# Two heads' last 64 keys as one square tile, and another order of the steps, in a linear-attention and mixing kernel

## The reference

```python
q_p, k_p = phi(q), phi(k)
kv = einsum('bhsf,bhsd->bhfd', k_p, v)      # sum over tokens
z = sum(k_p, axis=2)
out = (q_p @ kv) / (q_p . z + 1e-06)
```

## Time and profile before

| | us |
|---|---|
| median of three runs | 1393.31 |
| the three runs | 1392.87, 1393.31, 1397.05 |
| profiled execution, its own time | 1397.19 |
| its span, first to last instruction | 1395.3 |
| TensorE busy | 1333.8 |
| VectorE busy | 756.6 |
| ScalarE busy | 599.2 |
| mean granted TensorE clock | 0.981 |

### The profile page before, as it was taken

How to read it: one execution, slowest core, us unless ns; L and a number is a source line. 1 busy time by engine, 2 the same in 40 slices (tenths; PEclk the granted TensorE clock), 3 DMA queues, 4 the chain that set the end, 5 groups by cost and what they waited for, 6 DMA issues and landing times. The chain is left out here.

```text
span 1395.3 us, 25154 instructions
## 1 busy us (share of the span) xinstructions
PE 1333.8 (96%) x9720; PEld 1192.8 (85%) x9720; DVE 756.6 (54%) x1275; ACT 599.2 (43%) x1079; POOL 13.1 (1%) x18
## 2 busy tenths in 40 slices
PE   8779999999999999999999999998899999999998
PEld 7559898889888888888888888998798998998997
DVE  6557355545654544644565455451855755754853
ACT  3345445354353533534435344352533443533532
POOL 0000000000000000000000000000300000000000
PEclk9879999999999999999999999999999999999999
DMA  4421202202212111220221221221110110110101
GB/s 136 141 62 41 59 27 79 64 18 80 62 36 71 50 50 42 66 71 15 76 62 37 71 54 50 73 70 48 65 65 31 43 65 31 41 64 32 40 30 38
DMA packets 92657, 78.56 MB, mean 56 GB/s; under 512 B 62736, under 2 KB 71056, under 8 KB 91536
## 3 DMA queue, kind: packets, MB, share of 16 engines
q1 hardware_dynamic: 92560, 77.09, 18.4%
HBM read 57.75 MB, written 19.02 MB: 55 GB/s over the span
## 5 line engine op out<-in xcount | busy, mean ns | idle before, releaser
L459 PE MATMUL psm<-xk_hi,wk_hi 128*128 128x288 f32 x512 | 154.4, 302 | 14.5 <-issue 7.1
L982 PE MATMUL psh<-y_hi,win_hi 128*128 128x288 f32 x512 | 154.8, 302 | 13.4 <-ACT h L1067 9.0
L830 DVE TENSOR_TENSOR k_lo<-square,k_hi 128x288 fp32r<-128x288 f32 x128 | 58.5, 457 | 195.1 <-ACT square L677 194.8
L983 PE MATMUL psh<-y_lo,win_hi 128*128 128x288 f32 x512 | 153.1, 299 | 0.0
L459 PE MATMUL psm<-k_hi,wv_hi 128*128 128x288 f32 x512 | 152.8, 299 | 0.0
L984 PE MATMUL psh<-y_hi,win_lo 128*128 128x288 f32 x512 | 152.5, 298 | 0.0
L459 PE MATMUL psm<-xk_lo,wk_hi 128*128 128x288 f32 x512 | 152.2, 297 | 0.0
L459 PE MATMUL psm<-k_lo,wv_hi 128*128 128x288 f32 x512 | 152.0, 297 | 0.0
L459 PE MATMUL psm<-xk_hi,wk_lo 128*128 128x288 f32 x512 | 151.9, 297 | 0.0
L459 PE MATMUL psm<-k_hi,wv_lo 128*128 128x288 f32 x512 | 151.7, 296 | 0.0
L1125 DVE SCALAR_TENSOR_TENSOR conv<-h,taps,conv 128x576 f32<-128x576 f32 x64 | 55.2, 862 | 143.2 <-ACT conv L1069 143.2
(11 more groups left out here) (130 smaller groups left out, 2900.4 us busy)
## 6 DMA issues: line engine op xcount, KB each, us to landing
v_nat<-in_v SPq DMA_DIRECT2D x32, 320.0 KB, 3.6
qk<-in_q SPq DMA_DIRECT2D x32, 288.0 KB, 3.3
qk<-in_k SPq DMA_DIRECT2D x32, 288.0 KB, 3.7
den<-den_scr SPq DMA_DIRECT2D x64, 144.0 KB, 3.0
y_scr<-y SPq DMA_DIRECT2D x64, 144.0 KB, 2.0
y<-y_scr SPq DMA_DIRECT2D x8, 1152.0 KB, 5.6
out<-rows SPq DMA_DIRECT2D x32, 256.0 KB, 2.0
stage<-in_moe_w_in SPq DMA_DIRECT2D x4, 512.0 KB, 3.2
```

Source lines behind the costliest of these rows:

```text
L459: return nc.tensor.matmul(o, lhsT, rhs, start=first, stop=last, skip_group_check=True)
L830: nc.vector.tensor_tensor(k2_lo[:, i, :], square[:, i % 2, :], k2_hi[:, i, :].bitcast(F32), ALU.subtract).then_inc(k2_lo_ready, 1)
L982: nc.tensor.matmul(o, wh, xh, start=first, stop=False, skip_group_check=True)
L983: nc.tensor.matmul(o, wh, xl, start=False, stop=False, skip_group_check=True)
```

## The change

There are four parts. (1) The tails of both heads' keys become one square tile: the host lays k so that rows 0 to 63 hold head 0's last 64 tokens in columns 512 to 575 and rows 64 to 127 head 1's in columns 576 to 639, with zeros elsewhere, and v so that the tail tile holds head 0's tokens on partitions 0 to 63 and head 1's on 64 to 127. One matmul over 128 rows makes both tails' features, and one of 130 columns an exponential adds both heads' tails to the sums, which now lie as (exponential, head). (2) The second key exponential becomes a step of its own, EL. (3) The order: each batch's E(0) stands ahead of the tiles, RC, DV and the mixing steps stand at fixed places (`BESIDE_NEXT`, `ALONE`), VectorE takes each k_lo one tile later (`vector_order`), and HK and HR move from ScalarE to VectorE. (4) One iteration is taken out of the loop and written out, and pair 0's loads are issued during the iteration before.

```diff
+KEYS = 2 * (TT - 1) + 1
-FILL_NS = {"E": 1600, "QT": 1600, "EK": 3200, "PICK": 3200, "NUM": 1600}
-FIRST_FILL, RC_AFTER, DV_AFTER = 4000, 2500, 8500
+FILL_NS = {"E": 1600, "QT": 1600, "EK": 1600, "EL": 1600, "PICK": 3200, "NUM": 3200}
-    return [(s, p) for p in range(PAIRS) for s in ("E", "QT", "EK", "M", "KV", "PICK", "DEN", "NUM")]
+    return [(s, p) for p in range(PAIRS) for s in ("E", "QT", "EK", "EL", "M", "KV", "PICK", "DEN", "NUM")]
...
-        steps += [("E", p), ("QT", p), ("EK", p)] + before("DEN", "NUM") + [("WARM", p)] + before("RC")
-        steps += [("M", p), ("KV", p), ("PICK", p)] + before("DV")
+        steps += [("E", p), ("QT", p), ("EK", p), ("EL", p)] + ([("DV", p - 2)] if p > 1 else []) + before("DEN", "NUM") + [("WARM", p), ("M", p), ("KV", p)]
+        steps += before("RC") + [("PICK", p)]
     p = PAIRS - 1
-    steps += [("DEN", p), ("NUM", p), ("XK", 2, 0), ("HK", 2, 0), ("LK", 2, 0), ("RC", p)]
-    steps += [("XR", 2, 0), ("HR", 2, 0), ("LR", 2, 0), ("DV", p)]
-    return steps + [(s + w, 2, 1) for w in "KR" for s in "XHL"]
+    steps += [("DV", p - 1), ("DEN", p), ("NUM", p), ("RC", p)] + mixing("K", 2, 0) + mixing("R", 2, 0) + [("DV", p)]
+    return steps + mixing("K", 2, 1) + mixing("R", 2, 1)
...
+BESIDE_NEXT = {
+    ("M", 0): [("XK", 1, 0)],
+    ("QT", 1): [("RC", 0)],
+    ("M", 1): [("HK", 1, 0), ("LK", 1, 0)] + mixing("K", 1, 1) + mixing("R", 1, 0) + mixing("R", 1, 1) + [("DV", 0)],
+    ("QT", 2): [("RC", 1)],
+    ("PICK", 2): [("DV", 1)],
+    ("QT", 3): [("RC", 2)],
+    ("M", 3): [("DV", 2)] + mixing("K", 2, 0) + [("XR", 2, 0)],
+    ("R", 1, 3): [("HR", 2, 0), ("LR", 2, 0)],
+    ("V-", 1, 0): [("RC", 3)],
+    ("V", 1, 1): [("DV", 3)] + mixing("K", 2, 1) + mixing("R", 2, 1),
+}
...
+def vector_order(steps):
+
+    out, tile = [], []
+    for step in steps:
+        if step[0] in ("K", "K+", "R", "V"):
+            out += tile
+            tile = []
+        if step[0] in ("K", "K+"):
+            tile = [step]
+        else:
+            out.append(step)
+    return out + tile
...
-        with eng.Fori(1, LAST) as c:
+        with eng.Fori(1, LAST - 1) as c:
             work((c, 0), (c, 1), iteration(True, True))
+        work((None, LAST - 1), (None, LAST), iteration(True, True))
         work((None, LAST), None, iteration(True, False))
...
+                if kind == "E" and step[1] + 1 == PAIRS and after(a) is not None:
+                    load_qk(0, after(a))
                 if kind == "KV" and step[1] + 1 < PAIRS:
                     load_v(step[1] + 1, a)
+                if kind == "KV" and step[1] + 1 == PAIRS and after(a) is not None:
+                    load_v(0, after(a))
...
-            key_tile(0, TT - 1).then_inc(shared_bank, 1)
+            mm(k_tail(p, a), qk[:, p % 2, 1, P * (TT - 1):P * TT], phi[:], True, True).then_inc(shared_bank, 1)
             feature_chunk(1, 1, True)
             feature_chunk(0, 0, True)
-            await_(pe, shared_bank, 3 * PAIRS, a, 3 * p + 1)
-            key_tile(1, TT - 1).then_inc(shared_bank, 1)
-            key_tile(0, 0)
             key_tile(1, 0)
-            await_(pe, shared_bank, 3 * PAIRS, a, 3 * p + 2)
+            await_(pe, shared_bank, 2 * PAIRS, a, 2 * p + 1)
             feature_chunk(0, 1, True).then_inc(shared_bank, 1)
             key_tile(1, 1)
-            key_tile(0, 1)
-            await_(pe, shared_bank, 3 * PAIRS, a, 3 * p + 3)
+            key_tile(0, 0)
+            await_(pe, shared_bank, 2 * PAIRS, a, 2 * p + 2)
             feature_chunk(1, 0, False).then_inc(raw_features, 1)
-            for t in range(2, TT - 1):
-                for h in range(2):
-                    last = key_tile(h, t)
+            for h, t in ((0, 1), (1, 2), (0, 2), (1, 3), (0, 3)):
+                last = key_tile(h, t)
...
                 for h in range(2):
-                    for t in range(TT):
-                        last = mm(ps1[:, 0, VW * (2 * h + e):VW * (2 * h + e) + VW], src[:, h, t, :], v_nat[:, t, h, :],
-                                  t == 0, t == TT - 1)
+                    for t in range(TT - 1):
+                        at = VW * (2 * e + h)
+                        mm(ps1[:, 0, at:at + VW], src[:, (TT - 1) * h + t, :], v_nat[:, t, h, :], e == h == t == 0, False)
+                last = mm(ps1[:, 0, VW * 2 * e:VW * 2 * e + 2 * VW], src[:, KEYS - 1, :],
+                          v_nat[:, TT - 1, :, :].rearrange("p h n -> p (h n)"), False, e == 1)
...
-            nc.scalar.activation(hi[:, fs, :], mix[:, fs, :], ACT.Copy).then_inc(hi_ready, 1)
...
+            nc.vector.tensor_copy(hi[:, fs, :], mix[:, fs, :]).then_inc(hi_ready, 1)
```

More of the change, by code:

```diff
@@ L74, in iteration @@
+ALONE = {
+    ("R", 0, 0): mixing("K", 1, 0) + mixing("K", 1, 1),
+    ("R", 0, 3): mixing("R", 1, 0) + mixing("R", 1, 1),
+}
 def iteration(with_moe, with_next):
     tiles = []
-    for t in half_tiles(0) + half_tiles(1) if with_moe else []:
+    for t in half_tiles(0) + half_tiles(1):
         tiles += [("V-",) + t[1:], t] if t[0] == "V" else [t]
-    if with_moe:
-        tiles[0:3] = [("K-",) + t[1:] for t in tiles[0:3]] + [("K+",) + t[1:] for t in tiles[0:3]]
-    out, later, now, low_at = [], [], 0, {}
@@ L84, in mix @@
[L84 to L88, removed]
+    tiles[0:3] = [("K-",) + t[1:] for t in tiles[0:3]] + [("K+",) + t[1:] for t in tiles[0:3]]
+    beside = BESIDE_NEXT if with_next else ALONE
+    out = []
     def emit(step):
-        nonlocal now
         out.append(step)
[L93 to L102, removed]
+        out.extend(beside.get(step, []))
@@ L113, in iteration @@
     if with_next:
-        fill(FIRST_FILL)
         for step in attention_steps():
-            s, p = step[:2]
             emit(step)
[L118 to L127, removed]
+            fill(FILL_NS.get(step[0], 0))
     for u, t in enumerate(tiles):
@@ L339, in batches, with after @@
         work((None, 0), (None, 1), iteration(True, True))
-        with eng.Fori(1, LAST) as c:
+        with eng.Fori(1, LAST - 1) as c:
             work((c, 0), (c, 1), iteration(True, True))
+        work((None, LAST - 1), (None, LAST), iteration(True, True))
         work((None, LAST), None, iteration(True, False))
+    def after(a):
+        reg, off = a
+        return None if reg is None and off == LAST else (reg, off + 1)
     block = ctx.enter_context(nc.Block())
@@ L473, in features_and_keys @@
             await_(pe, k_loaded[p % 2], 16 * (PAIRS // 2), a, 16 * (p // 2 + 1))
-            tails, keys = k_tail(p, a), k_main()
+            keys = k_main()
             def key_tile(h, t):
                 own = slice(D * h, D * h + D)
-                o = tails[:, h, :] if t == TT - 1 else keys[:, h, t, :]
-                return mm(o, qk[own, p % 2, 1, P * t:P * t + P], phi[own, :], True, True)
+                return mm(keys[:, (TT - 1) * h + t, :], qk[own, p % 2, 1, P * t:P * t + P], phi[own, :], True, True)
             def feature_chunk(h, chunk, first):
@@ L700, in work @@
                     exp_k(step[1], a)
+                elif kind == "EL":
+                    exp_minus_k(step[1], a)
                 elif kind == "PICK":
@@ L841, in work @@
             pieces = 0
-            for step in steps:
+            for step in vector_order(steps):
                 kind = step[0]
@@ L1158 @@
         laid[name] = inputs[name].reshape(B, PAIRS, 2, S, D).transpose(0, 1, 2, 4, 3).reshape(B, PAIRS, 2 * D, S)
[L1159 to L1161 removed]
+    main = S - TAIL
+    tails = _np.zeros((B, PAIRS, 2, D, 2, TAIL), inputs["k"].dtype)
+    tokens = _np.zeros((B, PAIRS, P, TT, 2, D), inputs["v"].dtype)
+    heads = inputs["v"].reshape(B, PAIRS, 2, S, D)
+    tokens[:, :, :, 0:TT - 1] = heads[:, :, :, 0:main].reshape(B, PAIRS, 2, TT - 1, P, D).transpose(0, 1, 4, 3, 2, 5)
+    for h in range(2):
+        tails[:, :, h, :, h] = laid["k"].reshape(B, PAIRS, 2, D, S)[:, :, h, :, main:]
+        tokens[:, :, TAIL * h:TAIL * h + TAIL, TT - 1, h] = heads[:, :, h, main:]
+    laid["k"] = _np.concatenate([laid["k"][..., 0:main], tails.reshape(B, PAIRS, P, 2 * TAIL)], axis=-1)
+    laid["v"] = tokens.reshape(B, PAIRS, P, TT * 2 * D)
     for name in _INS:
```

73 lines of the change are left out of this document (33 added, 40 removed).

## The result

The kernel after the change takes 1346.96 us (four runs, 1346.06 to 1347.16) beside 1395.18 us for the kernel before (four runs, 1392.87 to 1400.32): a ratio of 0.9648 with a 95% interval of 0.9618 to 0.9678, 48.2 us less. The forecast was 1356 us and 37.5 us less. The sign, the bounds and the main mechanism were right. The time came out 9 us better than the likeliest value, and the saving 10.7 us larger, as the kernel before took 1395.18 us in these runs and not 1393.31.

What follows compares the result with a forecast made beforehand. TensorE, busy 1333.8 of 1395.3 us, was taken as the bound in the seven iterations. Savings of 12.3 + 2.8 + 9 + 1.9 + 1.5 + 10 = 37.5 us off 1393.3 gave about 1356 us, range 1343 to 1377.

Steps and rivals of the forecast that it cites:

- KV, 12.3 us: Key sums in the seven iterations: 18 matmuls instead of 20 save 0.44 us a pair over 28 pairs, 12.3 us.
- Rival 4: Key sums: the wide sum tile costs two narrow ones, so KV saves nothing, 1368 us; chance 0.03.
- E, 2.8 us: Features and keys: 13 matmuls instead of 14 and a new order save 0.1 us a pair, 2.8 us.
- Rival 3: In E the 128-row tail breaks the pairing of passes: 5.6 us lost instead of 2.8 won, 1364 us; chance 0.10.
- Waits for M, 9 us: In the iterations, TensorE's 14 waits for max_blocks go as M moves ahead of mixing and divide: 9 us saved.
- Rival 1: In the iterations, VectorE's added work keeps M late, so the waits stay: 1371 us; chance 0.15.
- Splits on VectorE, at nothing: HK and HR moved from ScalarE add 4.0 us an iteration to a half-idle VectorE; counted at nothing.
- Loop turn, 1.9 us: One iteration leaves the loop, so one turn less with its empty pipeline: 1.9 us saved.
- Loads, 1.5 us: The next batch's q, k and v load before the iteration's end, so the wait for k goes: 1.5 us saved.
- Start and seam, 10 us: First batch's attention and its seam to the iterations: RC's waits no longer delay M, net 10 us saved (5 to 14).
- Rival 2: The start turns its waits into others (num for x, XK for RC(3)): 3 us instead of 10, 1363 us; chance 0.12.
- Rival 5: Second key exponential comes late behind a tile's ScalarE work: 61.6 us lost over 28 pairs, slower at 1426 us; chance 0.03.

Runs made afterwards that it cites:

- tail_only: Kernel before with only the joined square tail, alternating heads inside E and KV's wide tile, order of steps as before: 1375.67 us, ratio 0.9879.
- order_only: Changed kernel with two separate tails again (E's 14 matmuls, KV's 20), everything else as changed: 1364.92 us, ratio 0.9802 to the kernel before.
- klo_direct: Changed kernel without the rule that VectorE takes k_lo one tile later: 1350.84 us, ratio 0.9704 to the kernel before.
- rc_early: Changed kernel with RC(0), RC(1), RC(2) one step earlier, behind E instead of QT of the next pair: 1345.53 us, ratio 0.9658 to the kernel before.
- h_scalar: Changed kernel with HK and HR back on ScalarE at the same steps: 1439.8 us, ratio 1.0319 to the kernel before.
- mix_first: Changed kernel with pair 1's mixing block and DV(0) ahead of M(1) instead of behind it: 1395.13 us, ratio 1.0028 to the kernel before.
- late_loads2: Changed kernel with pair 0's loads issued at the head of the iteration again, behind the y stores: 1387.49 us, ratio 0.9958 to the kernel before.
- late_looped2: As late_loads2, with the written-out seventh iteration put back into the loop, one loop turn more: 1388.02 us, ratio 0.9951 to the kernel before.

## Why the prediction was right, and where its terms were off

**KV, 12.3 us: right.** 28 x (4.39 - 3.94) = 12.6. The pass of 130 columns costs what the others do, within the 0.01 us that the earlier trace rows suggested. Rival 4 falls.

**E, 2.8 us: right in sign, too small.** 28 x 0.17 = 4.8 us, toward the better end. tail_only, where the steps kept their order, has the same 2.60. Three things changed inside E (a matmul less, heads that alternate, one wait for the shared bank less) and no run parts them; what is shown is that the 128-row tail doesn't cost more than they give. The Trainium skill (TensorEngine Tiling (Array Packing), Key Properties) says that a change of tiling mode drains TensorE. The trace doesn't contradict it: E is entered from 128-row passes and left into them in both kernels, so whatever a change of mode costs is paid as often as before. Rival 3 would have needed one more change, which a 128-row matmul at the very front doesn't make.

**Waits for M, 9 us: right, but half of a pair's wait was not seen.** From KV's second half to pick the kernel before lost 0.36 us a pair, 28 x 0.36 = 10.1. But TensorE also stood ahead of M, for q_part. In the kernel before that shows only among the weight loads' waits:

```profile
PEld ps L459 <- DVE max_blocks L782: 9.1, 14, 1.2
PEld ps L515 <- DVE q_part L770: 6.0, 21, 0.3
```

The prediction read the waits of PE's matmuls alone. The matmul that turns the maxima takes q_part as its weights, so the engine's wait is charged to the load. After has no such row. The lengths around M show what this was worth. In the kernel before, the last 12 passes ahead of M took 1.85, 1.59, 1.78 and 1.79 us in pairs 0 to 3 (medians), and in after 1.59 in each: the three pairs with a wait are the three that were longer. M took 0.06 us more on average, and KV's first half 0.06 more than its shortest. That is 0.6 + 4 x 0.06 + 4 x 0.06 = 1.1 us an iteration, 7.7 us in all, the largest part of what the forecast fell short by. What brought q_part in time isn't one thing: the waits of pair 2 go with tail_only alone (14 waits left, 4.1 us), order_only has none, klo_direct brings back those of pair 3 only (7, 1.7 us), and rc_early a single one (0.3 us). So RC's place behind QT did next to nothing for it. Rival 1, VectorE keeping M late, falls: M has 2.2 us of room in pair 1, as worked out.

**Splits on VectorE, at nothing: right for VectorE, but the wrong question.** A cast of 864 columns takes 0.61 us and one of 288 takes 0.31, against the estimates of 0.74 and 0.25. VectorE has room. What the move is worth lies on ScalarE: 93 us, by h_scalar, with the whole mixing behind M. The prediction costed where the work went and not what it would have blocked where it was.

**Loop turn, 1.9 us: right.** 109.2 us from E(0) to E(0) with a turn (four, on average) and 107.2 without: 2.0.

**Loads, 1.5 us: the size right, the weight wrong.** The old wait's 1.3 us is gone. But the part is a precondition: with E(0) in front and the loads left where they were, 40 us of the gain are lost.

**Start and seam, 10 us: 6.7 in this execution.** At pick(3) the walk's total came out: forecast "some 10.5 us cumulative", measured 79.87 before and 69.41 after. The links did not, and that is luck: pick(1) came at 34.57, not at 36.8, since the weights' split ended at 33.08 and not at 35.23, and in pairs 2 and 3 waits for max_blocks of 2.80 and 1.33 us were left, the first with the clock at half behind it. RC's waits no longer hold M:

```profile
31.86 1.22 DVE L743 TENSOR_TENSOR wk_lo<-mix,wk_hi 128x1024 fp32r<-128x1024 f32 x1 [1.20 <-ACT wk_hi L645]
33.00 0.28 DVE L772 TENSOR_REDUCE q_max<-psm 128x32 f32<-128x128 f32 x1
...
37.51 0.17 DVE L786 SCALAR_TENSOR_TENSOR den_cols<-den_parts 128x9 f32<-128x9 f32 x1 [0.18 <-DMA den_parts<-den_rows]
```

Behind it RC(3) came at 82.15 (forecast 81.4) and K's last input ended at 91.98 + 0.46 = 92.44 (forecast 91.5). The loss sits in the next link, on VectorE, ScalarE and TensorE:

```profile
93.75 0.28 DVE L748 TENSOR_REDUCE k_max<-ps 128x1 f32<-128x128 f32 x1
```

```profile
96.84 1.16 ACT L651 ACTIVATE k_exp<-k_shift 128x1152 f32<-128x1152 f32 x1 [16.74 <-issue]
97.91 0.39 ACT L682 ACTIVATE relu<-psm 128x288 f32<-128x288 f32 x1
```

```profile
98.35 0.40 PE L471 MATMUL psm<-xk_hi,wk_hi 128*128 128x288 f32 x1 [4.05 <-ACT relu L682]
```

VectorE reaches the keys of E(0) only after the mixing (93.75), so the exponential starts at 96.84. ScalarE idles for it, though K's first tiles are done, because their relus stand behind EK(0) in its order. TensorE runs out of banks and waits 4.05 us. The prediction did say that E(0) would come late and priced it at "about 3 us given back", through M(0). The way was another (M(0) isn't waited for at all, relu is), and with the low clock before and after it the price is some 5 us by estimate: K's 60 passes take 16.28 us there instead of 8.05, at a granted clock of 0.73. Pick(0) comes at 107.21 against 117.14, with two K tiles (3.2 us) fewer done: 6.7 us net, where 10 was forecast. This is one execution: rc_early and mix_first have the same start and the same two waits at the seam (5.33 us and 4.3 us), but pick(0) comes at 103.32 and 104.33 there, as the wait in pair 2 is 1.52 and 1.89 us instead of 2.80 and less time passes at the low clock. By those two the start gives 9.6 to 10.6 us, the forecast's 10. So the seam's wait is shown, while the size of this miss is not. Rival 2, a start that turns its waits into others, has its mechanism here in part.

**The low clock, not counted.** The two stretches of low clock in the iterations of before, put at some 2.8 us, have no twin after. About 1 us of them is in the 10.1 above as well, as KV's second half was longer there. In the six iterations behind the first, TensorE of after stops for nothing longer than a loop turn.

**The sum as measured.** 12.6 + 4.8 + 10.1 + 7.7 + 2.0 + 1.5 + 6.7 = 45.4 us, and 2.8 for the low clock makes 48.2, against 49.9 between the two profiled executions' spans; 1.7 us are not assigned, some 3 with the part that is counted twice. Rival 5, the second exponential late, didn't occur.

## What to carry to other kernels

A wait of the bound engine can be charged to its weight loads: read both lists before an order is priced. A part costed at nothing because it has cover is not shown to be worth nothing: here the splits' move and the early loads were priced at 0 and 1.5 us, and taking either away from the new order costs 93 or 40 us. When a step is moved in an engine's fixed order, ask of each engine what stands behind its wait: relu behind an exponential, the query exponentials behind the splits, M behind the mixing gave away 5, 93 and 48 us.

## What the runs showed of the hardware that was not expected

A wait of TensorE mostly costs more than its length. E takes 2.60 us behind busy passes, and 4.85 us behind the load's wait of 6.59 us. In the start of after, pick and E behind a wait of 2.80 us show the same:

```profile
51.43 1.65 PE L471 MATMUL ps<-max_blocks,pick 128*128 128x512 f32 x4 [2.80 <-DVE max_blocks L780]
52.88 0.63 PE L471 MATMUL psm<-phi,qk 128*128 128x128 f32 x2
```

Pick takes 52.88 - 51.43 = 1.45 us instead of 0.77. The Trainium skill (TensorE: Matmul & The Clock Gate, Part 1) says that the gate sets TensorE's clock by how busy it has been; the trace agrees in both cases, with a granted clock of 1.00 or 0.99 in the stretch before the wait and 0.50 behind it, the lower of the two levels. In mix_first 48 us were lost to 37.0 us of waiting, in h_scalar 93 to 57.3. But the surcharge doesn't come with every wait, nor by its length alone: behind 3.48 us of wait the clock was 0.65 once and 1.00 another time in h_scalar, and in rc_early the wait of 1.52 us in the start left it at 1.00. What decides between them, no run here shows.

And two delays at the same place don't add in full: the loop turn, 2.0 us by itself, adds some 1.3 us to a load's wait in the traces of late_loads2 and late_looped2. SP, which issues the load, takes the turn as well: from the end of the last y store to the issue of k it is 1.12 us with a turn and 0.61 without.
